# A new order of three engines in the first tile's first step, and VectorE for the second network's lower weight parts

## The reference

```python
scale = np.minimum(mag, 0.999) / (mag + 1e-06)          # mag = |a|
for t in range(S):                                      # S = 768
    new_re = ar * S_re - ai * S_im
    new_im = ar * S_im + ai * S_re
    S_re, S_im = new_re + k_t v_t^T, new_im
    y[t] = q_t @ S_re
x = y, heads side by side                               # 3072 x 384
xn = x / sqrt(mean(x * x) + 1e-6) * rms_g
x = (silu(xn @ w_gate) * (xn @ w_val)) @ w_out          # first network, 384 -> 1536 -> 384
h = x @ w_in
out = softplus(h) @ w_out2                              # second network, 384 -> 2048 -> 384
```

## Time and profile before

| | before |
|---|---|
| median of 3 runs | 1146.66 us |
| profiled execution | 1146.07 us, of it the span 1144.2 us |
| TensorE | 1065.6 us busy (93%) |
| VectorE, ScalarE, GpSimd | 650.9, 723.9, 251.7 us busy |
| mean granted TensorE clock | 0.995 of full speed |

### The profile page before, as it was taken

The page is one execution under the profiler, slowest core; times in us unless marked ns, Lnnn a source line. Parts: engine busy times, 40 slices in busy tenths (PEclk is TensorE's granted clock), DMA queues, the critical chain, the costliest instruction groups (busy, mean ns, idle before and its releaser), DMA issues.

```text
span 1144.2 us, 16983 instructions
## 1 busy us (share of the span) xinstructions
PE 1065.6 (93%) x5474; PEld 910.4 (80%) x5474; DVE 650.9 (57%) x2170; ACT 723.9 (63%) x1327; POOL 251.7 (22%) x259
## 2 busy tenths in 40 slices
PE   0577789999999999999999999989999999999997
PEld 0577778888888888888888877878888888888886
DVE  6999888888888988888886110221222213122211
ACT  5687656667666656666674434476666666676664
POOL 2122100010000101000100125633333333333332
PEclk9999989999999999999999999999999999999999
DMA  5888743444533533454444137510101001010000
GB/s 133 193 196 191 163 97 90 94 112 104 133 90 91 127 90 91 98 137 94 110 95 118 33 64 188 132 60 1 56 1 36 20 1 55 0 55 0 28 1 29
DMA packets 54322, 97.37 MB, mean 85 GB/s; under 512 B 9057, under 2 KB 30433, under 8 KB 54241
## 3 DMA queue, kind: packets, MB, share of 16 engines
q1 hardware_dynamic: 33504, 63.34, 18.5%
q0 software_dynamic: 15552, 25.96, 14.0%
q10 hardware_dynamic: 5184, 7.08, 2.2%
HBM read 49.02 MB, written 9.50 MB: 51 GB/s over the span
## 4 chain that ended last, share of the span: by engine, by line
PE 51%; issue 25%; POOL 11%; DVE 9%; ACT 2%; DMA 1%; POOLq 0%; SPq 0%; DVEq 0%; ACTq 0%
PE gbank L1492 25%; PE ybank L1492 12%; POOL pl L534 10%; DVE prep L892 4%; PE xbank L1521 3%; PE sbank L1509 3%; PE xbank L1520 3%; PE xbank L1524 2%; PE xbank L1500 1%; DVE pk L892 1%; DVE prep L926 1%; DMA pl<-hid 1%; PE sbank L1532 1%; ACT prep L575 1%; DMA a_in<-in_a 1%
## 5 line engine op out<-in xcount | busy, mean ns | idle before, releaser
L1492 PE MATMUL gbank<-xh,slab 128*128 128x512 f32 x1296 | 406.5, 395 | 2.5 <-ACT xh L619 1.5
L1492 PE MATMUL ybank<-ph,slab 128*128 128x512 f32 x1008 | 314.6, 393 | 5.5 <-ACT ytile L667 2.6
L1492 PEld LDWEIGHTS gbank<-xh,slab 128*128 128x128 f32 x1296 | 242.2, 190 | 51.5 <-ACT xh L619 1.7
L1492 PE MATMUL gbank<-xl,slab 128*128 128x512 f32 x648 | 254.1, 392 | 0.0
L1492 PEld LDWEIGHTS ybank<-ph,slab 128*128 128x128 f32 x1008 | 186.2, 188 | 43.7 <-issue 7.1
L1492 PE MATMUL ybank<-pl,slab 128*128 128x512 f32 x504 | 196.3, 389 | 0.0
L534 POOL TENSOR_TENSOR pl<-hid,ph 128x512 fp32r<-128x512 f32 x96 | 125.7, 1309 | 265.6 <-ACT ph L827 265.6
L1366 DVE SCALAR_TENSOR_TENSOR hid<-gbank,hid 128x512 f32<-128x512 f32 x72 | 49.8, 692 | 213.2 <-ACT hid L818 213.2
L511 POOL DMA_DIRECT2D pl<-hid x72 | 61.3, 852 | 484.1 <-ACT pl L660 476.2
L1492 PEld LDWEIGHTS gbank<-xl,slab 128*128 128x128 f32 x648 | 122.5, 189 | 26.4
L1492 PEld LDWEIGHTS ybank<-pl,slab 128*128 128x128 f32 x504 | 94.6, 188 | 20.1
(11 more groups left out here) (154 smaller groups left out, 1575.4 us busy)
## 6 DMA issues: line engine op xcount, KB each, us to landing
pl<-hid POOLq DMA_DIRECT2D x72, 256.0 KB, 3.7
mm<-pk SPq DMA_DIRECT2D x96, 144.6 KB, 3.2
a_in<-in_a SPq DMA_DIRECT2D x24, 384.0 KB, 3.7
kq_in<-in_kq SPq DMA_DIRECT2D x24, 384.0 KB, 3.4
ytile<-in_w ACTq DMA_DIRECT2D x36, 192.0 KB, 4.1
slab<-in_w POOLq DMA_DIRECT2D x36, 192.0 KB, 5.4
prep<-in_w SPq DMA_DIRECT2D x32, 192.0 KB, 2.6
v_in<-in_v SPq DMA_DIRECT2D x24, 192.0 KB, 3.5
```

What stands on the lines that cost most here:

```text
L1492: last = pe.matmul(out, slab[:, slot + part, cols], x, start=f, stop=l)
```

## The change

1. **Lead.** ScalarE copies half 0 of unit x's outputs before its part of preparation n, half 1 after it; VectorE adds half 0's state sum between `limits` and `scale`, instead of behind the third scan.
2. **First step.** ScalarE: the first `silu` before the copy of half 1 and before unit 4's sums of squares, which go behind the change of function table. VectorE: the lead's last two state sums go behind `limits` and behind `scale`; the second mask goes ahead of the third product. TensorE: the outputs of half 0 go between block 2's gate and value, and block 3's gate goes ahead of the transposition (it then is left out of step 1).
3. **Unit 23's transposition** (step 3 of tile 4, where no attention is left) goes ahead of `out_block` on TensorE, and its high part ahead of `hi` on ScalarE.
4. **Passage.** VectorE makes the second network's lower weight parts in place of GpSimd; the twelfth slot goes behind the first block's `exp_of` and `sp_of`; TensorE's one small sum for the flags goes behind the second network's first tile.
5. **End.** VectorE makes the last block's lower part; ScalarE copies bank 2.

```diff
@@ GpSimd
-            def w2_lo_of(slot):
...
+            for T in range(NT):
+                for f in range(F1):
+                    lo(T, f)
...
-            with pool.Fori(0, NT) as T:
+            with pool.Fori(0, NT - 1) as T:
                 for f in range(F2):
                     lo2(T, f)
+            for f in range(F2 - 1):
+                lo2(NT - 1, f)
@@ ScalarE, lead
+                if x is not None:
+                    lead_y_half(x, 0)
                 mid_w2(n)
                 mid_rest(n)
                 if x is not None:
-                    lead_y(x)
+                    lead_y_half(x, 1)
                     x_sums(x)
@@ ScalarE, step
                 if n == LEAD:
-                    lead_y(x)
-                    x_sums(x)
+                    lead_y_half(x, 0)
                     silu(0, 0)
-                if n is not None:
+                    mid_w2(n)
+                    lead_y_half(x, 1)
+                elif n is not None:
                     mid_w2(n)
...
-                if x is not None and T + i:
+                if x is not None:
                     x_sums(x)
...
                 if m is not None:
                     kt_copy(m, 1)
+                elif x is not None:
+                    xh_of(x, par, col, T)
@@ ScalarE, second network
                     exp_of(T, f)
+                    if first and f == 0:
+                        w2_hi_of(F1 - 1)
...
             act.activation(ytile[:, 0, :], ybank[0][:, :], ACT.Copy).then_inc(end_act, 1)
+            act.wait_ge(last_bank, NJ)
+            act.activation(ytile[:, 2, :], ybank[2][:, :], ACT.Copy).then_inc(end_act, 1)
@@ VectorE, step
-                if not T + i:
-                    state_add(m - 1, 1)
                 if n is not None:
                     newton(n)
                     inverse(n)
                     limits(n)
-                if m is not None and T + i:
+                if not T + i:
+                    lead_state(m - 1, 0)
+                elif m is not None:
                     state_add(m - 1, 1)
                 if n is not None:
                     scale(n)
                 if T is not None and T + i:
                     p_of(T, 3 * i)
+                if final and i:
+                    w2_lo_of(3 * i - 1)
+                if not T + i:
+                    lead_state(m - 1, 1)
...
+                if not T + i:
+                    mask(m, 1)
                 if T is not None:
                     p_of(T, 3 * i + 2)
+                if final:
+                    w2_lo_of(3 * i + 1)
@@ VectorE, lead
                     limits(n)
+                if x is not None:
+                    lead_state(x, 0)
@@ VectorE, end
+            dve.wait_ge(hi2_done, F2 * NT)
+            dve.tensor_tensor(pl[:, (F2 - 1) % 2, :], hid[:, (F2 - 1) % 2, :], ph[:, (F2 - 1) % 2, :].bitcast(F32),
+                              ALU.subtract).then_inc(last_low, 1)
@@ TensorE, first_step
                 gate_val(0, 2, 0, 0)
+                outputs(m, 0)
                 gate_val(0, 2, 0, 1)
-                outputs(m, 0)
                 out_block(0, 2)
                 kt_of(m, 1)
                 scores(m, 1)
+                gate_val(0, 3, 0, 0)
                 xt_of(x, m)
                 outputs(m, 1)
@@ TensorE, step
+                if m is None and x is not None:
+                    xt_of(x, m)
                 if T is not None:
                     out_block(T, 3 * i + 2)
-                if x is not None:
+                if m is not None and x is not None:
                     xt_of(x, m)
@@ TensorE, second network
+                if by_bank:
+                    pe.wait_ge(last_low, 1)
...
+            tile2(0, 0, first=True)
             pe.wait_ge(plain_min, 5)
             pe.matmul(sbank[0:1, 0:1], okmin[:, :], one[:, :], start=True, stop=True).then_inc(plain_sum, 1)
-            tile2(0, 0, first=True)
```

More of the change, by code:

```diff
@@ L499, in w1_lo @@
                                    accum_op=ALU.add).then_inc(w_lo if f < EARLY else w_lo_late, 16)
-            def w2_lo_of(slot):
-                q0 = sum(len(x) for x in W2_PLAN[:slot])
-                for i, (kind, f) in enumerate(W2_PLAN[slot]):
-                    at_ = w2_slot(kind, f)
-                    pool.wait_ge(w2_hi, q0 + i + 1)
-                    pool.tensor_tensor(slab[:, at_ + 1, :], stage2[:, i, :], slab[:, at_, :].bitcast(F32),
-                                       ALU.subtract).then_inc(w2_lo, 1)
             def lo(T, f):
@@ L511, in lo @@
                 pool.dma_start(pl[:, f % 2, :], hid[:, f % 2, :], accum_op=ALU.add).then_inc(lo_done[f % 2], 16)
-            def tile(T, last=False):
-                for i in range(UT):
-                    if last and i:
-                        w2_lo_of(3 * i - 1)
-                    lo(T, 3 * i)
-                    if last:
-                        w2_lo_of(3 * i)
-                    lo(T, 3 * i + 1)
-                    if last:
-                        w2_lo_of(3 * i + 1)
-                    lo(T, 3 * i + 2)
-                if last:
-                    w2_lo_of(F1 - 1)
             for f in range(F1):
@@ L529, in _ @@
             for T in range(NT):
-                tile(T, last=T == NT - 1)
+                for f in range(F1):
+                    lo(T, f)
             def lo2(T, f):
@@ L789, in tile @@
                         x2_split(0, 0)
-                if last:
-                    w2_hi_of(F1 - 1)
             act.preload_act_table_set(LN_EXP)
@@ L1149, in y_out, with w2_lo_of, step @@
                 dve.tensor_copy(ytile[:, 2, :], ybank[2][:, :]).then_inc(y_dve, 1)
-            def step(n, m, x, par=0, col=0, T=None, i=0):
-                if not T + i:
-                    state_add(m - 1, 1)
+            def w2_lo_of(slot):
+                q0 = sum(len(x) for x in W2_PLAN[:slot])
+                for i, (kind, f) in enumerate(W2_PLAN[slot]):
+                    at_ = w2_slot(kind, f)
+                    dve.wait_ge(w2_hi, q0 + i + 1)
+                    dve.tensor_tensor(slab[:, at_ + 1, :], stage2[:, i, :], slab[:, at_, :].bitcast(F32),
+                                      ALU.subtract).then_inc(w2_lo, 1)
+            def step(n, m, x, par=0, col=0, T=None, i=0, final=False):
                 if n is not None:
@@ L1257, in lead @@
                     limits(n)
+                if x is not None:
+                    lead_state(x, 0)
+                if n is not None:
                     scale(n)
@@ L1383, in tile2 @@
                     sp_of(T, f)
+                    if first and f == 0:
+                        w2_lo_of(F1 - 1)
                     if f == 5 and not end:
```

41 lines of the change are left out of this document (18 added, 23 removed).

## The result

| | before | after |
|---|---|---|
| median of 4 runs each, same chip | 1146.32 us | 1129.74 us (1128.88 to 1130.55) |
| ratio after/before | | 0.9855, 95% interval 0.9838 to 0.9872 |
| profiled execution, span | 1146.07, 1144.2 us | 1129.63, 1127.8 us |
| TensorE busy | 1065.6 us | 1061.1 us (94%) |
| VectorE, GpSimd busy | 650.9, 251.7 us | 665.8, 218.9 us |

What follows compares the result with a forecast made beforehand. VectorE bounds the lead; TensorE bounds the rest, with few waits and a clock drop in the first step. Terms 1.0 + 7.5 + 1.6 + 4.9 + 0.6 = 15.6 us off 1146.66 gave 1131.1 us; 8-in-10 range 1128.8 to 1136.0.

Steps and rivals of the forecast that it cites:

- Lead: VectorE's state sum of half 0, hidden ahead of `scale` in four passes: 1.0 us off, bounds 0 and 1.3.
- First step: First tile's first step: old TensorE waits go, new ones of 0.2, 1.0, 0.4 us; 7.5 us off, bounds 2.9 and 9.1.
- The granted clock: First step: clock expected to stay at its upper level, 1.00, saving the 4.65 us lost at 0.50.
- rival A: First step: the clock falls all the same, costing 4.65 us again, 1135.7 us; chance 0.11.
- Unit 23: Ahead of the last tile: earlier transposition removes the 1.47 us wait for the lower part; 1.6 us off, lower bound 0.
- Passage: Passage to the second network: shorter waits for `lo` DMAs and `y_out`, flags' sum moved; 4.9 us off in all.
- the lower parts: Passage: VectorE replaces GpSimd, so `lo` DMAs are issued earlier; 1.3 and 0.4 us off two TensorE waits.
- the slot: Passage: first `exp_of` runs ahead of slot 12, so the 2.57 us wait goes; 2.7 us off, lower bound 1.3.
- End: Kernel's end: VectorE's subtraction takes 0.69 us against GpSimd's 1.27, shortening TensorE's 0.86 us wait; 0.6 us off.
- B: First tile: ScalarE and VectorE lag TensorE, 3 us of the gain turn into waits, 1134.1 us; chance 0.09.
- D: Passage: DMAs late from traffic, slot 12 still holds `y_out`; 1.5 of 4.9 us left, 1134.5 us; chance 0.07.
- C: First step: late table load idles TensorE 1.5 us, clock stays low; slower than before, 1150.6 us; chance 0.02.

## Why the prediction was right

By its own steps. *Lead*, 1.0 us: +0.9 when undone, some 0.75 by the rows, inside the bounds of 0 and 1.3. The way there was wrong: I named passes 0.25 us shorter, and they are 0.05 shorter, because I had not followed ScalarE: from `scale` to `xh` it takes 12.1 us in both kernels (96.24 to 108.40, 95.61 to 107.73), and VectorE now waits for it. *First step*, 7.5 us: +7.5 when undone, 7.9 and 7.6 by the rows. The inner sizes were off in the safe direction: I had new waits of 0.2, 1.0 and 0.4 us and got 0.36 and 0.23 in the rows (the copy of the keys starts at 148.87, where I had 149.5); ahead of the second gate no wait is shown, though its start at 141.47 lies 0.2 us behind the pitch of the matmuls. *The granted clock* did stay up, which 4.65 of the 7.5 us hung on; the runs show that this was a nearer thing than I put it. I argued that 0.87 us left the clock up and 2.37 brought it down. With 0.88 us it stayed up once and fell once, and it fell behind 0.56 us in the second step. So rival A's mechanism is real, at another price: behind these waits a fall lost 1.7 us, and the 5.1 to 5.2 us for which A had 4.65 were seen in the first step only behind the 2.37 us. Had the walk been 1 us too kind at the transposition, 1.7 us would have been lost in some executions, and not A's time. *Unit 23*, 1.6 us: the wait of 1.47 came back whole; by time it was 2.4, and the profile has 0.7 of the scattered transfer besides. *Passage*, 4.9 us: +4.1 in the median of mixed runs, 3.8 without and 6.5 with a fall of the clock. Its parts: the lower parts 1.6 us for 1.3 + 0.4, the slot 2.38 us of wait for 2.7, and 4.2 by time, of which 1.7 is clock. The two add to 5.8 and not to 4.1, since the clock fell in most runs of the one and in two of five of the whole. The flags' 0.5 came back in no run. Here I had not counted the clock at all. *End*, 0.6 us: 0.62 in the rows.

The parts undone one by one give 0.9 + 7.5 + 2.4 + 4.1, and 0.6 from the rows: 15.5 us of the 16.6. Taken against the kernel before that ran beside each (1146.43 and 1145.88 us), the same four are 0.8, 7.3, 2.8 and 4.5, and the sum is 16.0. What is missing is no more than the spread of the medians; two things that point that way are the profile after without a wait for `pl`, worth 0.65 us, and a fall of the clock in the passage that the kernel before may have in some executions (its profile has none). The runs don't settle it. That the time came out 1.4 us under the likeliest 1131.1 is likewise explained by no single term. Of the rivals, B (lagging helpers) and D (no gain in the passage) are refuted by the rows, C by the table load that ended at 137.6.

## What to carry to other kernels

Undo-one-part runs gave back, within a microsecond, what the waits in the rows say, as long as the clock and the scattered transfer are added. So price a TensorE wait at its length plus a chance of a fall of the clock behind it: here 1.7 us behind waits of 0.56 to 2.55 us, 5.1 to 5.2 behind the 2.37 us of the first step. Look for it in several executions, since one profile shows only one throw. Compare the same stretch of instructions between profiles, from one instruction to another, before trusting medians: here that gave 44.97 to 45.07 us in every profile without an edit in it, where the medians scatter by a microsecond. And where three in-order queues feed each other, move the helper's instruction that releases the chain ahead of those that only fill time: without the clock, the helpers' orders were worth 2.0 us here and TensorE's own 0.1.

## What the hardware showed that I had not expected

- Behind the same wait the clock fell in some profiles and not in others: behind 0.88 us in one kernel of two, behind 0.56 us but not behind 0.61 us at the same place in another kernel, behind 2.38 and 2.55 us but not behind 2.57 in the kernel before. The runs of the kernel with the 2.55 us fall into two groups 2.5 us apart. And a fall had one of two prices: 1.7 us in five profiles (behind 0.56, 0.88, 1.93, 2.38 and 2.55 us), 5.1 to 5.2 us in three (behind 2.37 us twice, and in the lead of a kernel that was kept at work there). What decides is open.
- At the end of the lead the clock comes up at a moment that differs from profile to profile: between 134.5 and 138.8 us in twelve (by the durations of the matmuls), not needed in a thirteenth, which had it up before, but after 144 us in the fourteenth, whose TensorE had the same instructions up to 149 us. Why is open.
- The column of the granted clock reads 1.00 until its first change in each trace here. In the kernel after it says so for a stretch in which the matmuls run at half the pace:

```profile
130.00:135.00 5.00, 5.00 (x20) 4.42 (x21) 4.86 (x15) 4.09 (x12) 2.45 (x3) 1.00 0.67 110
```

```profile
132.10 1.20 PE L1497 MATMUL gbank<-xh,slab 128*128 128x512 f32 x2
...
139.12 0.70 PE L1497 MATMUL gbank<-xh,slab 128*128 128x512 f32 x2
```

The first two matmuls of block 0's gate take 1.20 us there, those of its value 0.70 later. In the kernel that was kept at work in the lead, the same stretch reads 0.50. Early in a trace the matmul's own duration tells the clock, and the column doesn't.
